# Attention and two expert layers in one kernel: rows turned earlier, rounding shared, and the last expert's width chosen at run time

## The chip, the cores and the metric

The kernel runs on one core of a Trainium2 chip. The metric is device time in microseconds (us), the median of 3 runs. The core has five instruction streams that work beside each other and meet at semaphores: TensorE (PE; its weight loads are listed as PEld), VectorE (DVE), ScalarE (ACT), GpSimd (POOL) and SyncE (SP), which issues most transfers.

## The reference, cut to what matters

```python
attn_out = _attn_ref(q, k, v)                    # 4 batches, 8 heads, 576 tokens, 64 wide, block-causal
x = attn_out.transpose(0, 2, 1, 3).reshape(B * S, H * D)     # 2304 tokens x 512
x = ((x @ w1) * (x @ w2)) @ w3 @ w_out                       # first expert layer, dense
logits = x @ w_gate                                          # second layer: each token picks 2 of 8 experts
noisy = logits + np.log1p(np.exp(x @ w_noise)) * noise
top2 = np.argpartition(-noisy, 2, axis=1)[:, :2]
for e in range(8):                                           # e_w1[e]: 512 x 1024, e_w2[e]: 1024 x 512
    h = np.maximum(x[mask] @ w1[e], 0.0)
    out[mask] += top2_w[mask, k, None] * (h @ w2[e])
```

The reference, evaluated on its own inputs (seed 0), gives the eight experts 607, 574, 540, 597, 592, 560, 591 and 547 rows.

## The kernel before, in words

Every float32 operand of a product is cut into a high part (rounded for TensorE) and a low part (what is left), and a product is made of three: high by high, low by high, high by low. ScalarE or GpSimd makes the high part, VectorE or GpSimd the low one.

The program has four phases: attention, the fusing of w3 and w_out, the dense layer with the choice of experts (`emit`), and the experts. Only the last and its seam are touched.

The experts' phase goes by **stretches** of at most 640 rows of one expert. Here each expert has one, so there are eight: the first is written out (`first_stretch`), the next six are turns of one loop (`Fori` in `through`), the last is written out again. A stretch has five tiles of 128 rows. For each, TensorE does this:

- **turn** a tile (`turn_x(g, j)`, L1573: four transposes of 128x128 out of `ex_rows` into the PSUM tile `ps_a`). ScalarE rounds the turned tile into `xT_high` (`high_x`, L1226), VectorE makes `xT_low` (`low_x`, L1341). There are two PSUM tiles for this (XS = 2), so the turn of tile j waits for `xT_low` of tile j-2.
- **first product** (`first_product(g, before, h, width)`, L1593): in two parts h of the rows. In the first stretch they are rows 0 to 383 and 384 to 639, later 0 to 255 and 256 to 639. Each part has 8 blocks of 12 matmuls (4 chunks, 3 products each). ScalarE makes `hT_high` with Relu, VectorE `hT_low`. In the six loop turns the second part is cut to the rows in use: 320, 352 or 384 columns, chosen from `widths_i` by three `pe.If` branches that stand one behind the other in the code. The last stretch always takes 384.
- **second product** (`second_product(g, before, j)`, L1617): per tile 24 matmuls of 128x512 into `ps_turn` or `ps_small`. VectorE scales the result into `y_tile` (`take_y`), and GpSimd sends it by an indirect accumulating transfer into `out` (`add_y`, L1196).

Weights of the next expert arrive in raw form by SP's queue (`spare` for the first matrix, `w_raw` for the second, 1 MB a piece, two pieces each). GpSimd cuts each piece into high (`cut_high`, L1148) and low (`cut_low`, L1154), and counts `weights_cut`; TensorE waits for 4 counts before the next stretch's first product, SP waits for the counts to load the next raw piece.

Only the first stretch has another order, since its rows come late. Tiles 0 to 2 (AHEAD = 3) are turned at the end of the dense layer; tiles 3 and 4 can only be loaded when the last rows have been scattered. Then `plan_experts` on VectorE computes the stretches, GpSimd's `know_rows` reads the token numbers and weights, and SP loads the next stretch's rows (`ex_rows`) behind four raw weight pieces (L1078) on its one queue. The order within each engine is the order in which its functions are written; semaphores alone tie the engines.

Of the kernel before, what the change touches and what calls it, by code (L numbers as in the profile page):

```python
# [5 lines left out]
F32 = mybir.dt.float32  # L6
F32R = mybir.dt.float32r
ALU = mybir.AluOpType
# [848 lines left out]
def gated_product_and_experts(nc, xT, parts, w_gate_noise, noise, consts, C, store, spare, ahead, plan, w1, w2, w1_raw, places):  # L857
# [30 lines left out]
    XS, HS, YS = 2, 4, 2  # L888
    CUTS = 2 * PIECES
    READS = 11  # L890

    with ExitStack() as ctx:  # L892
        def sb(name, shape, dt=F32):
# [96 lines left out]
        second_high = sem("second_high")  # L990
        second_low = sem("second_low")
        weights_cut = sem("weights_cut")
        x_loaded = [sem(f"x_loaded{j}") for j in range(TILES)]
        ex_turned = sem("ex_turned")
        xhigh = sem("xT_high_ready")
# [134 lines left out]
        def _(pool):  # L1130
# [60 lines left out]
            def add_y(g, j):  # L1191
                pool.wait_ge(y_taken, TILES * g + j + 1)
                if j == 0:
# [2 lines left out]
                nc.gpsimd.indirect_dma_start(out=out, out_offset=bass.IndirectOffsetOnAxis(ap=out_rows[:, j:j + 1], axis=0),  # L1196
                                             in_=y_tile[j][:], in_offset=None, compute_op=ALU.add).then_inc(y_added[j], 16)

            def stretch(g, before, last):
                if before is not None:  # L1200
                    pool.wait_ge(y_done, TILES * g)
                    for k in range(PIECES, 2 * PIECES):
                        cut_high(g, k)
                        cut_low(before, k)
                know_rows(g, before)
                if last:
                    for j in range(TILES):
                        add_y(g, j)
                    return
                pool.wait_ge(h_done, UNITS * (g + 1))  # L1210
                cut_high(g + 1, 0)
                cut_low(g, 0)
                add_y(g, 0)
                cut_high(g + 1, 1)
                add_y(g, 1)
                cut_low(g, 1)
                for j in range(2, TILES):
                    add_y(g, j)
# [4 lines left out]
        def _(act):  # L1223
# [16 lines left out]
            def first_stretch():  # L1240


                high_x(0, 2)
                route(GROUPS - 1, 2)
                route(GROUPS - 1, 3)
                second_high_part(0)
                high_h(0, 0, PARTS_FIRST)
                second_high_part(1)
                high_h(0, 1, PARTS_FIRST)
                route(GROUPS - 1, 5)  # L1250
                second_high_part(2)
                high_h(0, 2, PARTS_FIRST)
                second_high_part(3)
                for q in range(3, FC):
                    high_h(0, q, PARTS_FIRST)
                for j in range(AHEAD, TILES):
                    high_x(0, j)
                for q in range(FC, UNITS):
                    high_h(0, q, PARTS_FIRST)
                for j in range(TILES):  # L1260
                    high_x(1, j)

            def stretch(g, before, last):
# [69 lines left out]
        def _(dve):  # L1333
# [30 lines left out]
            def first_stretch():  # L1364
# [22 lines left out]
                    take_y(0, None, j)  # L1387
                for q in range(FC, UNITS):
                    low_h(0, q, PARTS_FIRST)
                take_y(0, None, AHEAD - 1)  # L1390
                for j in range(AHEAD, TILES):
                    take_y(0, None, j)
                    for k in (range(AHEAD) if j == AHEAD else range(AHEAD, TILES)):
                        low_x(1, k)

            def stretch(g, before, last):
# [141 lines left out]
        def _(pe):  # L1538
# [61 lines left out]
            def second_product(g, before, j):  # L1600
# [9 lines left out]
                for f in range(FC):  # L1610
                    for h in range(len(parts)):
                        if rows.start == parts[h].start:
                            pe.wait_ge(hlow, UNITS * g + FC * h + f + 1)
                    if before is None and j == 0 and f % (FC // QUARTERS) == 0:
                        pe.wait_ge(second_low, f // (FC // QUARTERS) + 1)
                    for lhsT, rhs in ((hT_high, ew2_high), (hT_high, ew2_low), (hT_low, ew2_high)):
                        mm = nc.tensor.matmul(ps_y[j % YS][:], lhsT[:, f, rows], rhs[:, f], start=(n == 0), stop=(n == 3 * FC - 1))  # L1617
                        n += 1
                    if before is None and j == 1 and f >= FC - (TILES - AHEAD):
                        turn_x(0, f - FC + TILES)  # L1620
                mm.then_inc(y_done, 1)

            def first_stretch():

                first_product(0, None, 0)
                second_product(0, None, 0)
                second_product(0, None, 1)
                first_product(0, None, 1)
                second_product(0, None, 2)
                second_product(0, None, 3)  # L1630
                for j in range(AHEAD):
                    turn_x(1, j)
                second_product(0, None, 4)
                for j in range(AHEAD, TILES):
                    turn_x(1, j)

            def stretch(g, before, last):
                if before is None:
                    return first_stretch()
                pe.wait_ge(weights_cut, 2 * CUTS * before + CUTS)  # L1640
                first_product(g, before, 0)
                if last:
                    first_product(g, before, 1)
                else:
                    step = pe.value_load(widths_i[0:1, bass.ds(g, 1)], min_val=0, max_val=len(WIDTHS) - 1)
                    for k, width in enumerate(WIDTHS):
                        with pe.If(step == k):
                            first_product(g, before, 1, width)
                pe.wait_ge(weights_cut, 2 * CUTS * before + 2 * CUTS)
                for j in range(TILES):  # L1650
                    second_product(g, before, j)
# [284 lines left out]
```

## Time and profile before

| | us |
|---|---|
| median of 3 runs | 1051.24 (1050.34 to 1051.44) |
| the profiled execution | 1052.73 |
| its span (first to last instruction) | 1050.6 |
| TensorE busy | 1019.5 (97% of the span) |
| GpSimd busy | 540.7 (51%) |
| VectorE busy | 443.0 (42%) |
| ScalarE busy | 365.1 (35%) |

A share of busy time is a mean over all phases. Whether one engine's wait costs anything is read from TensorE: it is idle in very few places, and each row below marked with `[idle before <-releaser]` is one of them. All times in rows are microseconds from the span's start.

### The profile page before, as it was taken

How to read it: one execution, taken by the hardware profiler on the slowest of the kernel's cores; microseconds unless marked ns; L12 is line 12 of the kernel's file. 1: busy time of each engine (PE TensorE's matmuls, PEld its weight loads, DVE VectorE, ACT ScalarE, POOL GpSimd, SP SyncE). 2: the span in 40 equal slices, each digit the busy share in tenths (PEclk: the TensorE clock that was granted, in tenths of full speed). 3: DMA queues.
4: the chain of work that ended last, by engine and by line, in shares of the span. 5: the costliest groups of instructions: out<-in, count | busy, mean ns of one | idle time of the engine just before them, and what ended most of it. 6: DMA issues, size and time to landing. Idle time of an engine off the chain costs nothing.

```text
span 1050.6 us, 16706 instructions
## 1 busy us (share of the span) xinstructions
PE 1019.5 (97%) x5927; PEld 937.4 (89%) x5928; DVE 443.0 (42%) x935; ACT 365.1 (35%) x679; POOL 540.7 (51%) x426
## 2 busy tenths in 40 slices
PE   7999999898999999999999999999999999999996
PEld 5999999787989898989898988889898989898995
DVE  5788888664224243333325742222222223222211
ACT  5999888753212232222223411212121212111110
POOL 8688899530000202020202229968778787878742
PEclk8999999999999999999999999999999999999998
DMA  8788887293970101010402165362717163634303
GB/s 168 169 199 191 202 205 175 69 269 100 369 281 2 60 0 60 0 60 0 140 1 85 48 250 126 92 167 67 192 37 213 20 195 65 190 70 140 41 4 47
DMA packets 73681, 125.25 MB, mean 119 GB/s; under 512 B 13073, under 2 KB 30609, under 8 KB 73634
## 3 DMA queue, kind: packets, MB, share of 16 engines
q1 hardware_dynamic: 64594, 103.74, 34.1%
q0 software_dynamic: 8960, 20.61, 9.9%
q8 instruction: 28, 0.46, 0.2%
q10 hardware_dynamic: 80, 0.29, 0.1%
q14 instruction: 19, 0.16, 0.1%
HBM read 78.73 MB, written 36.67 MB: 110 GB/s over the span
## 4 chain that ended last, share of the span: by engine, by line
PE 72%; POOL 1%; DVE 1%; issue 1%; ACT 0%; POOLq 0%; DVEq 0%
PE ps_turn L1617 11%; PE ps_b L1593 10%; PE ps_x L1593 10%; PE ps_a L1670 9%; PE ps_x L1688 9%; PE ps_b L1670 9%; PE ps_small L1617 8%; PE ps_a L1573 1%; PE ps_small L1565 1%; PE ps_turn L1555 1%; POOL w_high L1148 1%; POOL w_low L1154 1%; POOL out L1196 0%; PE ps_small L1547 0%; POOLq L892 0%
## 5 line engine op out<-in xcount | busy, mean ns | idle before, releaser
L1139 POOL DMA_INDIRECT expert_rows<-x_rows,slot_idx x36 | 41.7, 1159 | 307.5 <-DVE slot_idx L1493 298.4
L1196 POOL DMA_INDIRECT out<-y_tile,out_rows x40 | 63.3, 1581 | 77.1 <-DVE y_tile L1357 72.4
L1226 ACT CAST xT_high<-ps_a 128x512 fp32r<-128x512 f32 x40 | 23.3, 587 | 197.3 <-PE ps_a L1573 197.3
L1593 PE MATMUL ps_b<-xT_high,w_high 128*128 128x256 f32 (+3 forms) x256 | 78.0, 305 | 2.1 <-DVE xT_low L1341 1.4
L1294 ACT COPY prod<-ps_a 128x384 f32<-128x384 f32 x48 | 23.0, 479 | 163.7 <-PE ps_b L1670 163.7
L1500 DVE TENSOR_TENSOR prod<-ps_b,prod 128x384 f32<-128x384 f32 x48 | 26.7, 557 | 125.5 <-ACT prod L1294 125.5
L1617 PE MATMUL ps_turn<-wo_high,hT_high 128*128 128x512 f32 x192 | 76.2, 397 | 1.4 <-DVE hT_low L1348 1.4
L1593 PE MATMUL ps_x<-xT_high,w_high 128*128 128x256 f32 (+3 forms) x256 | 77.3, 302 | 0.0
L1593 PE MATMUL ps_x<-xT_high,w_low 128*128 128x256 f32 (+3 forms) x256 | 77.2, 302 | 0.0
L1593 PE MATMUL ps_x<-xT_low,w_high 128*128 128x256 f32 (+3 forms) x256 | 77.2, 302 | 0.0
L1593 PE MATMUL ps_b<-xT_high,w_low 128*128 128x256 f32 (+3 forms) x256 | 77.2, 302 | 0.0
L1593 PE MATMUL ps_b<-xT_low,w_high 128*128 128x256 f32 (+3 forms) x256 | 77.2, 302 | 0.0
L1617 PE MATMUL ps_turn<-wo_high,hT_low 128*128 128x512 f32 x192 | 75.0, 391 | 0.0
L1617 PE MATMUL ps_turn<-wo_low,hT_high 128*128 128x512 f32 x192 | 74.9, 390 | 0.0
L306 DVE TENSOR_TENSOR pT_low<-work,pT_high 128x512 fp32r<-128x512 f32 (+2 forms) x112 | 68.1, 627 | 11.1 <-ACT work L390 10.6
L1148 POOL TENSOR_TENSOR w_high<-spare,consts 128x2048 fp32r<-128x2048 f32 x14 | 54.3, 3882 | 33.0 <-PE ps_x L1593 33.0
L1670 PE MATMUL ps_a<-x_high,w_high 128*128 128x384 f32 x192 | 66.5, 347 | 2.8 <-DVE x_low L1527 2.8
L1154 POOL TENSOR_TENSOR w_low<-spare,w_high 128x2048 fp32r<-128x2048 f32 x14 | 68.4, 4888 | 0.5
L389 ACT ACTIVATE pT_high<-work 128x512 fp32r<-128x512 f32 (+2 forms) x112 | 62.1, 555 | 9.8 <-PE work L528 9.3
L1154 POOL TENSOR_TENSOR wo_low<-w_raw,wo_high 128x2048 fp32r<-128x2048 f32 x14 | 64.8, 4627 | 1.1
L1670 PE MATMUL ps_a<-x_high,w_low 128*128 128x384 f32 x192 | 64.9, 338 | 0.0
L1670 PE MATMUL ps_a<-x_low,w_high 128*128 128x384 f32 x192 | 64.8, 337 | 0.0
(269 smaller groups left out, 3024.4 us busy)
## 6 DMA issues: line engine op xcount, KB each, us to landing
spare<-e_w SPq DMA_DIRECT2D x16, 1024.0 KB, 5.2
w_raw<-e_w SPq DMA_DIRECT2D x16, 1024.0 KB, 8.7
expert_rows<-zeros SPq DMA_DIRECT2D x8, 1290.0 KB, 15.1
ex_rows<-expert_rows SPq DMA_DIRECT2D x40, 258.0 KB, 4.4
k_raw<-kT SPq DMA_DIRECT2D x31, 288.0 KB, 4.9
out<-zeros SPq DMA_DIRECT2D x11, 512.0 KB, 10.6
q_raw<-qT SPq DMA_DIRECT2D x16, 288.0 KB, 5.4
q_mix<-q_top SPq DMA_DIRECT2D x16, 288.0 KB, 3.8
```

The costliest lines, as they stand in the source:

```text
L306: nc.vector.tensor_tensor(unit_of(pT_low, unit), unit_scores(unit), unit_of(pT_high, unit).bitcast(F32), ALU.subtract)\
L389: nc.scalar.activation(unit_of(pT_high, unit), unit_scores(unit), ACT.Exp, scale=SCALE).then_inc(high_done, 1)
L1139: nc.gpsimd.indirect_dma_start(out=rows_dram, out_offset=bass.IndirectOffsetOnAxis(ap=slot_idx[:, k, t:t + 1], axis=0), in_=x_rows[:, t, : ...
L1148: nc.gpsimd.tensor_tensor(high, loaded, zero.unsqueeze(2).to_broadcast(list(loaded.shape)), ALU.add)\
L1154: nc.gpsimd.tensor_tensor(low, loaded, high.bitcast(F32), ALU.subtract).then_inc(weights_cut, 1)
L1196: nc.gpsimd.indirect_dma_start(out=out, out_offset=bass.IndirectOffsetOnAxis(ap=out_rows[:, j:j + 1], axis=0), in_=y_tile[j][:], in_offset ...
L1226: nc.scalar.copy(xT_high[:, :, j * P:(j + 1) * P], ps_xT[j % XS][:].rearrange("p (c t) -> p c t", t=P)).then_inc(xhigh, 1)
L1500: nc.vector.tensor_tensor(prod[f % 2][:], ps_b[f % 2][:, 0:G], prod[f % 2][:], ALU.mult).then_inc(prod_done, 1)
L1593: mm = nc.tensor.matmul(ps_hT[q % HS][:, 0:rows.stop - rows.start], lhsT[:, c, f * P:(f + 1) * P], rhs[:, c, rows], start=(n == 0), stop=( ...
L1617: mm = nc.tensor.matmul(ps_y[j % YS][:], lhsT[:, f, rows], rhs[:, f], start=(n == 0), stop=(n == 3 * FC - 1))
L1670: mm = nc.tensor.matmul(ps[f % 2][:, 0:G], lhsT[:, c, f * P:(f + 1) * P], rhs[:, c], start=(n == 0), stop=(n == 3 * DC - 1))
L1688: mm = nc.tensor.matmul(ps_x[t % 2][:], lhsT[:, f, t * P:(t + 1) * P], rhs[:, f], start=(n == 0), stop=(n == 3 * FC - 1))
```

## The change

Five edits, all in the experts' phase:

1. In the second product of tile 1 of the first stretch, the turns of tiles 3 and 4 stand behind blocks 3 and 4 (of 0 to 7), where they stood behind 6 and 7.
2. The five turns of the next stretch's tiles in the first stretch stand as 2, 2 and 1 behind the second products of tiles 2, 3 and 4; they stood as 3 and 2 behind tiles 3 and 4. VectorE's `low_x` follows the same table.
3. ScalarE rounds the two pieces of the next first weights, between the second and the third turned tile; GpSimd's two `cut_high` of that place are gone and it makes the low parts only.
4. GpSimd issues the output transfers of tiles 0 and 1 before these low parts, where the first stood behind the first piece and the second in the midst of the second.
5. The last stretch chooses its width by the same three branches as the loop turns.

```diff
+    LATE_TURNS = (3, 4)
+    NEXT_TURNS = {2: (0, 1), 3: (2, 3), 4: (4,)}
...
+            def first_stretch():                     # GpSimd
+                know_rows(0, None)
+                for j in range(AHEAD - 1):
+                    add_y(0, j)
+                for k in range(PIECES):
+                    loaded, high, low = piece(k)
+                    pool.wait_ge(next_high, k + 1)
+                    nc.gpsimd.tensor_tensor(low, loaded, high.bitcast(F32), ALU.subtract).then_inc(weights_cut, 2)
+                for j in range(AHEAD - 1, TILES):
+                    add_y(0, j)
...
-                for j in range(TILES):               # ScalarE
+                for j in NEXT_TURNS[AHEAD - 1]:
+                    high_x(1, j)
+                for k in range(PIECES):
+                    loaded, high, _ = piece(k)
+                    act.wait_ge(raw_loaded[k], 16)
+                    act.wait_ge(h_done, UNITS)
+                    nc.scalar.copy(high, loaded).then_inc(next_high, 1)
+                for j in range(len(NEXT_TURNS[AHEAD - 1]), TILES):
                     high_x(1, j)
...
-                take_y(0, None, AHEAD - 1)           # VectorE
-                for j in range(AHEAD, TILES):
+                for j in range(AHEAD - 1, TILES):
                     take_y(0, None, j)
-                    for k in (range(AHEAD) if j == AHEAD else range(AHEAD, TILES)):
+                    for k in NEXT_TURNS[j]:
                         low_x(1, k)
...
-                    if before is None and j == 1 and f >= FC - (TILES - AHEAD):     # TensorE
-                        turn_x(0, f - FC + TILES)
+                    if before is None and j == 1 and f in LATE_TURNS:
+                        turn_x(0, AHEAD + LATE_TURNS.index(f))
...
-                second_product(0, None, 2)
-                second_product(0, None, 3)
-                for j in range(AHEAD):
-                    turn_x(1, j)
-                second_product(0, None, 4)
-                for j in range(AHEAD, TILES):
-                    turn_x(1, j)
+                for j in range(AHEAD - 1, TILES):
+                    second_product(0, None, j)
+                    for k in NEXT_TURNS[j]:
+                        turn_x(1, k)
...
-                if last:
-                    first_product(g, before, 1)
-                else:
-                    step = pe.value_load(widths_i[0:1, bass.ds(g, 1)], min_val=0, max_val=len(WIDTHS) - 1)
-                    for k, width in enumerate(WIDTHS):
-                        with pe.If(step == k):
-                            first_product(g, before, 1, width)
+                step = pe.value_load(widths_i[0:1, bass.ds(g, 1)], min_val=0, max_val=len(WIDTHS) - 1)
+                for k, width in enumerate(WIDTHS):
+                    with pe.If(step == k):
+                        first_product(g, before, 1, width)
```

What this does to the streams is shown at three places. First GpSimd, from the end of `know_rows` (L1189) to the end of the first stretch; L1148 is a high part, L1154 a low part, L1196 an output transfer. Before:

```order
L1189 CAST out_rows<-row_of 128x5 [waits rows_read]
L1148 TENSOR_TENSOR w_high<-spare,consts 128x2048 [waits raw_loaded0,h_done]
L1154 TENSOR_TENSOR w_low<-spare,w_high 128x2048 [waits weights_cut]
L1196 DMA out<-y_tile_4238,out_rows 2944x512 [waits y_taken,rows_known]
L1148 TENSOR_TENSOR w_high<-spare,consts 128x2048 [waits raw_loaded1]
L1196 DMA out<-y_tile_4239,out_rows 2944x512 [waits y_taken]
L1154 TENSOR_TENSOR w_low<-spare,w_high 128x2048 [waits weights_cut]
L1196 DMA out<-y_tile_4240,out_rows 2944x512 [waits y_taken]
```

And now (L1199 is the transfer, L1210 the low part):

```order
L1192 CAST out_rows<-row_of 128x5 [waits rows_read]
L1199 DMA out<-y_tile_4238,out_rows 2944x512 [waits y_taken,rows_known]
L1199 DMA out<-y_tile_4239,out_rows 2944x512 [waits y_taken]
L1210 TENSOR_TENSOR w_low<-spare,w_high 128x2048 [waits next_high] x2
L1199 DMA out<-y_tile_4240,out_rows 2944x512 [waits y_taken]
```

The two high parts have left this stream, the first two transfers no longer wait for the first product's end (h_done), and the other three still stand behind both low parts.

Second, ScalarE at the same place, now (before, one row `xT_high<-ps_a` x5 stood where the last four rows stand; L1248 is `high_h`, L1242 `high_x`, L1282 the new rounding):

```order
L1248 ACTIVATE hT_high<-ps_b 128x256 [waits h_done] x2
L1248 ACTIVATE hT_high<-ps_x 128x256 [waits h_done] x2
L1242 CAST xT_high<-ps_a 128x4x128 [waits ex_turned] x2
L1282 CAST w_high<-spare 128x2048 [waits h_done,raw_loaded0]
L1282 CAST w_high<-spare 128x2048 [waits h_done,raw_loaded1]
L1242 CAST xT_high<-ps_a 128x4x128 [waits ex_turned] x3
```

The third turned tile now queues behind both roundings.

Third, TensorE. The end of the second product of tile 1 (`ps_small`, three matmuls to a block) before, with the first product's second part behind it:

```order
L1617 MATMUL ps_small<-wo_high,hT_low 128x512
L1573 MATMUL ps_a<-consts,ex_rows 128x128 x4
L1617 MATMUL ps_small<-wo_high,hT_high 128x512
L1617 MATMUL ps_small<-wo_low,hT_high 128x512
L1617 MATMUL ps_small<-wo_high,hT_low 128x512
L1573 MATMUL ps_a<-consts,ex_rows 128x128 x4
L1593 MATMUL ps_b<-xT_high,w_high 128x256
```

Now the same two turns have a block between them and more of the second product behind:

```order
L1595 MATMUL ps_a<-consts,ex_rows 128x128 x4
L1639 MATMUL ps_small<-wo_high,hT_high 128x512
L1639 MATMUL ps_small<-wo_low,hT_high 128x512
L1639 MATMUL ps_small<-wo_high,hT_low 128x512
L1595 MATMUL ps_a<-consts,ex_rows 128x128 x4
L1639 MATMUL ps_small<-wo_high,hT_high 128x512
```

And the end of the narrowest branch of the last stretch, now (before, this part was straight code of 96 matmuls of 128x384):

```order
L1615 MATMUL ps_x<-xT_high,w_high 128x320
L1615 MATMUL ps_x<-xT_high,w_low 128x320
L1615 MATMUL ps_x<-xT_low,w_high 128x320
L1663 UNCONDITIONAL_BRANCH
L1663 COMPARE_AND_BRANCH
L1601 REGISTER_ALU
L1605 REGISTER_ALU
L1615 MATMUL ps_b<-xT_high,w_high 128x352
```

Behind it stand the 96 matmuls of 352 columns and the 96 of 384, each jumped over when not chosen, and then the second product.

## Rows read from the trace of the kernel before

**Rows 1.** Waits of TensorE, 570 to 1051 us (line, releaser: total us, times, longest).
```profile
PE ps_b L1593 <- DVE xT_low L1341: 1.4, 1, 1.4
PE ps_turn L1617 <- DVE hT_low L1348: 1.4, 1, 1.4
PE ps_a L1573 <- DVE xT_low L1341: 1.1, 1, 1.1
```

**Rows 2.** Timeline of TensorE around the late turns: start, us, instruction, [idle before].
```profile
608.48 0.39 PE L1617 MATMUL ps_small<-wo_high,hT_high 128*128 128x512 f32 x1
...
614.37 0.60 PE L1573 MATMUL ps_a<-consts,ex_rows 128*128 128x128 f32 x4
616.37 0.39 PE L1593 MATMUL ps_b<-xT_high,w_high 128*128 128x256 f32 x1 [1.40 <-DVE xT_low L1341]
```

**Rows 3.** Timeline of TensorE at the end of the first stretch.
```profile
633.46 0.39 PE L1617 MATMUL ps_small<-wo_high,hT_high 128*128 128x512 f32 x1
...
638.90 1.04 PE L1573 MATMUL ps_a<-consts,ex_rows 128*128 128x128 f32 x8
640.99 0.63 PE L1573 MATMUL ps_a<-consts,ex_rows 128*128 128x128 f32 x4 [1.05 <-DVE xT_low L1341]
641.38 0.48 PE L1617 MATMUL ps_turn<-wo_high,hT_high 128*128 128x512 f32 x1
...
648.64 0.38 PE L1593 MATMUL ps_b<-xT_high,w_high 128*128 128x256 f32 x1 [0.67 <-POOL w_low L1154]
```

**Rows 4.** Timeline of GpSimd, 631 to 649 us.
```profile
631.92 4.61 POOL L1154 TENSOR_TENSOR w_low<-spare,w_high 128x2048 fp32r<-128x2048 f32 x1
...
643.24 5.15 POOL L1154 TENSOR_TENSOR w_low<-spare,w_high 128x2048 fp32r<-128x2048 f32 x1
```

**Rows 5.** ScalarE's casts by form (count, busy us, mean ns, idle before).
```profile
L760 ACT CAST w_high<-spare 128x1024 fp32r<-128x1024 f32 x8 | 8.4, 1052 | 1.8 <-DMA spare<-w 1.8
...
L1322 ACT CAST x_high<-xT 128x1536 fp32r<-128x1536 f32 x1 | 1.5, 1476 | 0.0
```

**Rows 6.** Issues in windows 606.9:608, 618:618.2, 636:637 (count, KB, us to landing).
```profile
ex_rows<-expert_rows SPq DMA_DIRECT2D x2, 258.0 KB, 2.9
...
ex_rows<-expert_rows SPq DMA_DIRECT2D x1, 258.0 KB, 9.5
...
out<-y_tile,out_rows POOLq DMA_INDIRECT x1, 6.5
```

**Rows 7.** Windows (busy per engine, PEclk); the last two columns are DMA share and GB/s.
```profile
616.00:618.00 2.00, 1.63 (x13) 1.63 (x14) 1.63 (x3) 0.00 (x0) 0.00 (x0) 1.00 1.02 418
...
642.00:648.00 6.00, 5.97 (x31) 4.80 (x29) 1.44 (x2) 0.67 (x2) 5.83 (x3) 1.00 0.45 62
```

**Rows 8.** Chain that ended last, whole span: start, us, what.
```profile
616.37 3.14 PE ps_b L1593 x24
...
657.53 2.88 PE ps_x L1593 x24
660.41 3.52 PE ps_b L1593 x24
...
670.97 3.53 PE ps_x L1593 x24
675.84 5.74 PE ps_turn L1617 x24
...
727.76 3.52 PE ps_x L1593 x24
731.28 5.47 PE ps_turn L1617 x24
...
1009.36 4.16 PE ps_x L1593 x24
1013.52 5.48 PE ps_turn L1617 x24
```

**Rows 9.** DMA queues, window 672:674 (queue: packets, MB, share).
```profile
q8 instruction: 1, 0.02, 4.2%
```

More of the change, by code:

```diff
@@ L992, in gated_product_and_experts @@
         weights_cut = sem("weights_cut")
+        next_high = sem("next_high")
         x_loaded = [sem(f"x_loaded{j}") for j in range(TILES)]
@@ L1197, in add_y @@
                                              in_=y_tile[j][:], in_offset=None, compute_op=ALU.add).then_inc(y_added[j], 16)
-            def stretch(g, before, last):
[L1200 to L1204, printed above, removed]
+            def first_stretch():
[8 more added lines that the diff above has]
+                    add_y(0, j)
+            def stretch(g, before, last):
+                if before is None:
+                    return first_stretch()
+                pool.wait_ge(y_done, TILES * g)
+                for k in range(PIECES, 2 * PIECES):
+                    cut_high(g, k)
+                    cut_low(before, k)
                 know_rows(g, before)
```

## Prediction

> **What bounds the kernel now.** I read the waits first. In the experts' phase TensorE is idle at four places that concern this change [rows 1, 3]; elsewhere its matmuls follow one another, and over the whole span it is busy for 97% (the page's table). So a gain must be one of these waits, or fewer columns on TensorE. Then I read the timelines around each wait, to see who ends it and who comes next, then the other engines and the queues there, and last the chain through the second, the third and the last stretch.
>
> The waits: (a) 1.40 us before 616.37, where the first product's second part waits for `xT_low` of tile 4, turned just before [rows 2]; (b) 1.05 before 640.99, where the third turn in a row waits for a PSUM tile [rows 3]; (c) 0.67 before 648.64, where the second stretch waits for GpSimd's last low part [rows 3]; (d) 1.34 between 674.50 (670.97 + 3.53) and 675.84, before the second product of the second stretch [rows 8]. The profile puts (d) down to `hT_low`, but the second product of tile 0 needs only the first part's rows, whose `hT_low` is long done. It occurs in the first loop turn alone: in the next one 727.76 + 3.52 = 731.28 is exactly where the second product starts [rows 8]. In the window just before it a packet of instructions is fetched [rows 9]. I read (d) as code that had not arrived: after the 320-column branch the program jumps over two bodies of 96 matmuls each.
>
> **Edit 1, the late turns.** Before, the last late turn starts at 614.37 and the product that needs it at 616.37: the way turn, ScalarE, VectorE, TensorE takes 2.00 us [rows 2]. A second product of 24 matmuls takes 638.90 - 633.46 = 5.44 us [rows 3], so a block of three takes 0.68. The second product of tile 1 starts at 608.48 [rows 2]; the first late turn now starts after four blocks, at 611.2, the second after one turn (0.44: four transposes of the eight in 1.04, less the overlap) and one block, at 612.3, and its result is usable at 614.3. TensorE ends this second product at 614.97 as before (614.37 + 0.60). So (a) goes whole, 1.40. What could be late instead is the rows: tiles 3 and 4 come by two issues near 607 that land after 2.9 us, at 609.9 [rows 6], and the turn comes 1.3 us later. A product that starts after a wait also fills slowly: the first 24 matmuls took 3.14, unbroken ones 2.88 [rows 8], so 0.26 more. I count 1.66; bounds 0 (the rows late by that much) and 1.66.
>
> **Edit 2, the next turns.** No more than two turns stand together, so none waits for a PSUM tile: (b) goes, 1.05. One more change between kinds of matmul costs 0.48 - 0.39, about 0.1, the first matmul behind a turn against one in the row [rows 3]. The turns are five, as before.
>
> TensorE's new calendar, if nothing waits: the first product's second part from 614.97, four times 2.88, to 626.5; second product of tile 2 to 632.0; two turns to 632.9; tile 3 to 638.4; two turns to 639.3; tile 4 to 644.9; one turn to 645.35. Then the next stretch starts, if its weights are cut.
>
> **Edits 3 and 4, the weights.** GpSimd's second low part ended at 643.24 + 5.15 = 648.39 [rows 4], and TensorE started 0.25 behind it. Now ScalarE rounds the first two turned tiles (from 632.0, done at 633.7) and then the two pieces. The trace has no ScalarE cast of 128x2048. 128x1024 took 1.052 and 128x1536 took 1.476 [rows 5]; on that line 2048 columns take 1.90. Bounds: 1.5 (no shorter than 1536 columns) and 2.1 (twice 1024). GpSimd starts its first low part at 635.6, takes 4.61, and the second ends at 644.85; with 5.15 for each [rows 4] it ends at 645.9. TensorE wants it at 645.35. So (c) goes, 0.67 and the slow fill 0.26, together 0.93, less 0 to 0.8. What is late next is this same low part, by a margin of nothing. Queued behind the two roundings on ScalarE is the third turned tile: ScalarE is free again at 637.5, and that tile is turned only at 638.4. VectorE's `low_x` and `take_y` have TensorE's calendar, and TensorE needs them next for the turn of tile 4 at 644.9. Queued behind the low parts on GpSimd are the transfers of tiles 2 to 4, which leave from 645 on where they left from 648.4 on: nobody waits longer. SP loads the next raw piece into `spare` behind the first low part, at 640.2 instead of 636.5 (631.92 + 4.61), and GpSimd reads it only when the second stretch's first product is through, past 670: hidden.
>
> Moved past others are the two output transfers. They now go out at 616 to 618 and meet SP's queue, where four raw pieces and then the rows of the next stretch are under way with all 16 DMA engines full (share 1.02, 418 GB/s) [rows 7]. The first tile of these rows is issued at 618.1 and lands 9.5 us later, at 627.6 [rows 6]. It was wanted at 638.9 and is now wanted at 632.0: the slack falls from 11.3 to 4.4. An output transfer issued at 642.2 stands nearly alone in the window 642 to 648, 0.45 x 6 = 2.7 us of all engines [rows 7]. Two are 5.4: in the worst order tile 0 lands at 633.0 and tile 1 some 0.8 later, wanted at 632.4, a wait of up to 1.4. In the best order they take nothing that the rows need: 0. I take 0.2 for this and for the margin above together.
>
> The DMA page says that each DMA engine goes round between the queues it has work for, packet by packet (Trainium skill, DMA: Bandwidth & Descriptors, Queues, rings and completion order). By that rule the two transfers get through beside SP's queue, what they take falls on what is last there, the rows, and the sum would be 1.2 us smaller than mine; no row here shows the two together.
>
> **Edit 5, the width.** The last expert has 547 rows by the reference, so 320 columns. In the last stretch 24 matmuls of 384 columns take 4.16, in the loop 24 of 320 take 3.52 [rows 8]; there are four such groups, 4 x 0.64 = 2.56 less. But this code was straight: the second product started without a gap, at 1009.36 + 4.16 = 1013.52 [rows 8]. Now it has the loop's jumps, in code met for the first time. The one first time that the trace shows is (d): 1.34, and a slow restart of 5.74 - 5.47 = 0.27 [rows 8]. It is the same branch, 320 columns with two bodies jumped, so I charge 1.61. Bounds: 0 (the code is there) and 3.2 (both jumps wait). The load of the width's register in the second stretch cost nothing: 657.53 + 2.88 = 660.41 is where the part begins [rows 8]. ScalarE and VectorE get the loop's pace, and the last transfers follow TensorE's end as before.
>
> The launch page says that a taken jump whose target is outside the fetched window forces a fetch before execution goes on (Trainium skill, Runtime: NRT & Kernel Launch, Instruction fetch mechanics). The trace agrees in (d). The page also says that only straight fetching is served, by which every loop turn would pay; the third stretch pays nothing [rows 8], and there the trace decides.
>
> **The sum.** First stretch: 1.66 + 1.05 - 0.10 + 0.93 - 0.20 = 3.34. Last: 2.56 - 1.61 = 0.95. Together 4.3. Against the profiled execution, 1052.73 - 4.3 = 1048.4; that one lies 1.5 above the median of the runs. For the median: 1051.24 - 4.3 = **1046.9**. The gap (d) itself stays: as many instructions stand ahead of it as before.
>
> **Rivals.**
>
> *The branch is free.* If the fetched code is already there, the last stretch keeps its 2.56: 1046.9 - 1.6 = 1045.3. For it: the third stretch jumps without a gap. Against it: its code had run before.
>
> *The branch gives nothing.* Each of the two jumps waits in full, 3.2 against 2.56: 1051.24 - 3.34 + 0.65 = 1048.6. For it: two jumps, each to code not yet run. Against it: in (d) two jumps cost 1.6 together. The launch page's rule, taken jump by jump, is this case.
>
> *The rows or the low part are late.* 1.4 us at the turn or 0.8 at the low part, of which 0.2 is counted: 1047.5 to 1048.1. For it: full DMA engines and a margin of nothing. Against it: 4.4 us of slack.
>
> *Slower.* The mechanism is the two early output transfers. They read and add in memory; if, on full engines, they go one after the other and hold up the rows for their whole time to landing, 6.5 us each as the one of 636.7 [rows 6], the first tile lands at 627.6 + 13 = 640.6. Its turn is 8.6 late, the second stretch starts at 645.35 + 8.6 = 654.0 instead of 648.64, and with 0.95 from the last stretch the kernel takes 1051.24 + 5.3 - 0.95 = 1055.6. It decides once the rows are delayed by more than 4.4 + 3.3 + 0.95 = 8.6 us. Against it: 2.7 us of engine time each.
>
> **Chances.** Forecast 0.55; branch free 0.14; branch gives nothing 0.09; rows or low part late 0.14; slower 0.04; all else 0.04. A measurement of this kernel can tell about 0.2%, 2.1 us, from no change, so faster means below 1049.1: the first four, less the cases where two losses meet, 0.88. Within 0.2%: 0.08. Slower: 0.04. The range, 1045.0 to 1049.4, holds the first four with their unknown costs and leaves out the slower case.
>
> **What would show it.** Right: no wait at the start of the first product's second part near 615, none between turns; the second stretch starting near 645.3 instead of 648.64, with a few tenths at most waited for the low part; ScalarE's new casts near 1.9 each; 24 matmuls of 320 columns in 3.52 in the last stretch, and 1.3 to 1.4 us of gap before its second product. Wrong: a turn that waits for `ex_rows` near 632, the second stretch starting after 647, or a gap in the last stretch of nothing or near 3.

## The result, and the profile after

| | before | after |
|---|---|---|
| median of the runs | 1051.34 us (1050.34 to 1052.70, 4 runs) | 1045.44 us (1044.77 to 1045.93, 4 runs) |
| ratio | | 0.9937, 95% interval 0.9919 to 0.9954 |
| profiled execution (span) | 1052.73 (1050.6) | 1045.19 (1043.0) |

By the ratio the kernel is faster by 6.6 us (4.8 to 8.5), where 4.3 were forecast; the two medians differ by 5.9. The ratio times 1051.24 is 1044.6, just under the low end of the range, 1045.0.

The two spans differ by 7.6 us. The first stretch's first product starts at 585.82 before and at 584.67 after, so 1.15 us lie in phases that the change does not touch. That start fell anywhere between 582.6 and 589.8 us in the kernels below. I therefore measure every kernel from that start, by the starts of TensorE's matmuls in its timeline. A runs from there to the second stretch's first product; B from there to its second product; C is the same as B in the last stretch; "all" is the way to the last matmul.

| kernel | A | B | C | all |
|---|---|---|---|---|
| before | 62.82 | 27.20 | 28.23 | 454.56 |
| after | 59.10 | 27.09 | 25.67 | 448.14 |
| after less before | -3.72 | -0.11 | -2.56 | -6.42 |

Of the waits at [rows 1, 3], the two for `xT_low` and the one for GpSimd's `w_low` are gone. The one put down to `hT_low` stays. Waits of TensorE after the change, 570 to 1051 us (columns as in rows 1):

```profile
PE ps_turn L1639 <- DVE hT_low L1371: 1.2, 1, 1.2
PE ps_small L1587 <- DVE w_raw L1545: 0.8, 1, 0.8
PE ps_turn L1577 <- ACT x_rows L1339: 0.2, 1, 0.2
```

The timeline of TensorE after the change answers to [rows 2, 3]: the two late turns, the first product's second part, the first two next turns and what follows them, the start of the second stretch.

```profile
610.05 0.60 PE L1595 MATMUL ps_a<-consts,ex_rows 128*128 128x128 f32 x4
...
611.19 0.60 PE L1595 MATMUL ps_a<-consts,ex_rows 128*128 128x128 f32 x4
...
613.72 0.28 PE L1615 MATMUL ps_b<-xT_high,w_high 128*128 128x256 f32 x1
...
630.69 1.03 PE L1595 MATMUL ps_a<-consts,ex_rows 128*128 128x128 f32 x8
631.48 0.48 PE L1639 MATMUL ps_small<-wo_high,hT_high 128*128 128x512 f32 x1
...
643.77 0.38 PE L1615 MATMUL ps_b<-xT_high,w_high 128*128 128x256 f32 x1
```

No bracket stands behind any of these: TensorE is never idle before them. The second part now starts 613.72 - 584.67 = 29.05 behind A's start; before it was 616.37 - 585.82 = 30.55. The second stretch starts at 643.77, which on the clock of before (1.15 later) is 644.92, where 645.35 was forecast. Two turns take 631.48 - 630.69 = 0.79 from start to start. Before, the two turns with the wait (b) behind them took 640.99 - 638.90 = 2.09 [rows 3], so (b) had cost 1.30: its 1.05 and a slow restart of 0.25.

ScalarE and GpSimd after the change, in the same stretch, answer to [rows 4]:

```profile
632.29 3.73 ACT L1282 CAST w_high<-spare 128x2048 fp32r<-128x2048 f32 x2
...
615.82 1.70 POOL L1199 DMA_INDIRECT out<-y_tile,out_rows  x1 [1.71 <-DVE y_tile L1380]
617.83 1.58 POOL L1199 DMA_INDIRECT out<-y_tile,out_rows  x1 [0.31 <-issue]
634.36 9.17 POOL L1210 TENSOR_TENSOR w_low<-spare,w_high 128x2048 fp32r<-128x2048 f32 x2 [14.95 <-ACT w_high L1282]
```

The two casts take 1.87 each and the two low parts 9.17 together. GpSimd ends at 643.53, and TensorE starts 0.24 later. Before, where it did wait for the low part, it started just as long behind it (648.39 and 648.64). So the margin of nothing that was forecast is what the trace shows, and yet no wait is seen.

The chain of waits after the change, in the second and in the last stretch (start, us, what), answers to [rows 8]:

```profile
666.10 3.53 PE ps_x L1615 x24
...
670.86 5.74 PE ps_turn L1639 x24
...
1002.46 3.52 PE ps_x L1615 x24
1005.98 5.46 PE ps_turn L1639 x24
```

In the second stretch 666.10 + 3.53 = 669.63, and the second product starts 1.23 later. In the last one 1002.46 + 3.52 = 1005.98 is exactly where the second product starts. The width branch runs there at the pace of 320 columns, and the gap that I had charged for it is not there.

### The profile page after: what moved, and what is told of

It is laid out like the page before. It is cut to its first block, busy times and chain, and to the rows that moved or that the text cites. A ratio compares the mean times of both kernels' runs of the same rounds, so it can differ in the third digit from the quotient of the medians.

```text
span 1043.0 us, 16716 instructions
## 1 busy us (share of the span) xinstructions
PE 1014.5 (97%) x5927; PEld 933.6 (90%) x5928; DVE 443.0 (42%) x935; ACT 368.3 (35%) x681; POOL 533.9 (51%) x424
## 4 chain that ended last, share of the span: by engine, by line
PE 74%; DVE 1%; ACT 0%; POOLq 0%; issue 0%; DVEq 0%
PE ps_turn L1639 13%; PE ps_x L1615 10%; PE ps_b L1615 10%; PE ps_a L1686 10%; PE ps_x L1704 9%; PE ps_b L1686 9%; PE ps_small L1639 8%; PE ps_a L1595 2%; PE ps_small L1587 1%; PE ps_turn L1577 1%; PE ps_small L1569 0%; POOLq L894 0%; PE ps_small L1570 0%; DVE y_tile L1380 0%; DVE w_raw L1545 0%
## 5 line engine op out<-in xcount | busy, mean ns | idle before, releaser
L1199 POOL DMA_INDIRECT out<-y_tile,out_rows x40 | 63.3, 1581 | 76.1 <-DVE y_tile L1380 71.5
L1242 ACT CAST xT_high<-ps_a 128x512 fp32r<-128x512 f32 x40 | 23.3, 587 | 190.3 <-PE ps_a L1595 190.3
L1686 PE MATMUL ps_b<-x_high,w_high 128*128 128x384 f32 x192 | 64.4, 335 | 0.0
L1686 PE MATMUL ps_b<-x_low,w_high 128*128 128x384 f32 x192 | 64.3, 335 | 0.0
```

Of the source, the lines that this page charges most:

```text
L1242: nc.scalar.copy(xT_high[:, :, j * P:(j + 1) * P], ps_xT[j % XS][:].rearrange("p (c t) -> p c t", t=P)).then_inc(xhigh, 1)
L1686: mm = nc.tensor.matmul(ps[f % 2][:, 0:G], lhsT[:, c, f * P:(f + 1) * P], rhs[:, c], start=(n == 0), stop=(n == 3 * DC - 1))
```

## The experiments

The first stretch first, then the code fetch. The whole time of a single execution is of little use (the phases ahead scatter by more than the effects), so what is said of each kernel rests on A, B and C of one trace; only the changed kernel, no_branch and pad_both have a ratio of several runs too. A short table at the end has them all.

**late_only.** Before, with the two late turns as changed.

```diff
-                    if before is None and j == 1 and f >= FC - (TILES - AHEAD):
-                        turn_x(0, f - FC + TILES)
+                    if before is None and j == 1 and f in LATE_TURNS:
+                        turn_x(0, AHEAD + LATE_TURNS.index(f))
```

> The kernel before with edit 1 alone (late turns behind blocks 3 and 4). Theory: the wait of 1.40 us before the first product's second part goes with its slow fill, and GpSimd's cuts, which start at the end of that product, start as much earlier. From the first stretch's first product to the second stretch's it is 62.67 us before; expected 61.0 (1.66 less). Waits of 1.05 (third turn) and about 0.7 (low part) stay. Rival (the rows of tiles 3 and 4 or GpSimd hold it up): nothing gained, 62.7.

A is 61.20, 1.62 less than before, against a term of 1.66. The other two waits of the first stretch stand as they were, in the waits of TensorE of this kernel:

```profile
PE ps_a L1575 <- DVE xT_low L1343: 1.1, 1, 1.1
PE ps_turn L1619 <- issue: 1.0, 1, 1.0
...
PE ps_b L1595 <- POOL w_low L1156: 0.7, 1, 0.7
```

The term of edit 1 is as forecast. The gap (d) is in the list too, 1.0 long, and here the profile names no releaser for it but "issue".

**turns_only.** The late turns and the spread next turns (edits 1 and 2), with the weights and the transfers as before.

```diff
+    NEXT_TURNS = {2: (0, 1), 3: (2, 3), 4: (4,)}
```

> The kernel before with edits 1 and 2 (late turns, next turns spread), the weights cut by GpSimd with the transfers in between as before. My prediction's terms were added up: by them 62.67 - 1.66 - 1.05 + 0.10 = 60.06 us from first product to first product. Theory now: GpSimd's second low part is the bound (it ended at 648.39 and is only 1.66 earlier), so 61.0, with the wait for the low part grown to about 1.6; edit 2 alone gains nothing.

A is 61.17: the spread turns add 0.03 to edit 1 alone, although the wait between turns is gone. The waits of TensorE in this kernel:

```profile
PE ps_b L1594 <- POOL w_low L1156: 1.9, 1, 1.9
```

What was waited for a PSUM tile is now waited for GpSimd: 0.7 has become 1.9. GpSimd's calendar hadn't moved, and TensorE merely came earlier to the same release.

**no_scalar.** After, without ScalarE's rounding: GpSimd rounds and subtracts itself, as before, but with the two transfers ahead of all its pieces (edit 3 undone, edit 4 kept).

```diff
+                pool.wait_ge(h_done, UNITS)
                 for k in range(PIECES):
-                    pool.wait_ge(next_high, k + 1)
-                    nc.gpsimd.tensor_tensor(low, loaded, high.bitcast(F32), ALU.subtract)...
+                    cut_high(1, k)
+                    cut_low(0, k)
```

> The changed kernel with edit 3 undone: GpSimd cuts both pieces itself (high and low), but the first two transfers stay ahead and nothing lies between the cuts. Theory: what freed the path is the two transfers' removal, not ScalarE's rounding. GpSimd starts at the end of the first product and takes 3.60 + 4.61 + 3.60 + 4.61 and small gaps, 16.6 us, so it ends 2 us before TensorE's second stretch wants it: 59.15 us from first product to first product as in the changed kernel, no wait for the low part. Rival (ScalarE's rounding is needed): GpSimd's parts take 4.2 and 5.2 as in the crowded place, 18.8 us, and TensorE waits 0.3 to 1.

A is 59.07, the same as after within 0.03. Timeline of GpSimd in this kernel:

```profile
627.72 3.60 POOL L1151 TENSOR_TENSOR w_high<-spare,consts 128x2048 fp32r<-128x2048 f32 x1 [6.03 <-PE ps_x L1610]
631.39 4.61 POOL L1157 TENSOR_TENSOR w_low<-spare,w_high 128x2048 fp32r<-128x2048 f32 x1
...
639.63 4.60 POOL L1157 TENSOR_TENSOR w_low<-spare,w_high 128x2048 fp32r<-128x2048 f32 x1
```

GpSimd alone ends at 639.63 + 4.60 = 644.23; TensorE starts the second stretch at 646.00 in this kernel, so the low part ends 1.8 ahead of that, where ScalarE's help leaves 0.2. From the start of the first piece to the end of the last GpSimd takes 644.23 - 627.72 = 16.51 here; before, with two output transfers between the pieces, it took 648.39 - 628.24 = 20.15. These 3.6 us had made it late. Given edit 4, edit 3 takes nothing off the time, and it narrows the margin. Edit 3 with the transfers in their old places was not run.

**no_spread.** After, with the turns where they were before.

```diff
-    NEXT_TURNS = {2: (0, 1), 3: (2, 3), 4: (4,)}
+    NEXT_TURNS = {2: (), 3: (0, 1, 2), 4: (3, 4)}
```

> The changed kernel with edit 2 undone: the next turns stand as 3 and 2 again, ScalarE rounds the pieces ahead of all of them. Theory: the wait of 1.05 us for a PSUM tile at the third turn is back, 60.1 us from first product to first product (59.15 + 1.05 - 0.10). Rival (the wait was only the other side of GpSimd's lateness): 59.2.

A is 60.60, 1.50 more than after. The wait between turns is back with 1.06, and with it 0.25 of slow restart: from the two turns to the third it is 641.34 - 639.24 = 2.10 on TensorE's timeline, against 0.79 for two turns without a wait. The other 0.2 lies just ahead of the second stretch and stays open. So edit 2 is worth 1.5 with edits 3 and 4 in place, and 0.03 without them. By no_scalar edit 4 is the one of the two that counts: edits 2 and 4 are one gain that needs both parts.

**transfers_late.** After, with all five output transfers behind the low parts.

```diff
-                for j in range(AHEAD - 1):
-                    add_y(0, j)
...
-                for j in range(AHEAD - 1, TILES):
+                for j in range(TILES):
                     add_y(0, j)
```

> The changed kernel with edit 4 undone, farther than before: all five output transfers stand behind both low parts (ScalarE still rounds). Theory: the two transfers cost the next rows 2.8 us (time to landing of the first 9.5 again, where the changed kernel has 12.3), but the rows are not waited for, so 59.1 us from first product to first product as in the changed kernel. Rival (my prediction's, that the transfers can hold up the turn): shorter than 59.1.

A is 59.09, as after. What counts is that no transfers stand between GpSimd's pieces; whether they leave early or last is the same. They do take the rows' time. Issues of DMA in this kernel, window 621:622.2 (count, KB, us to landing):

```profile
ex_rows<-expert_rows SPq DMA_DIRECT2D x1, 258.0 KB, 9.4
```

And the issues of the same rows in the changed kernel, window 616:617.2:

```profile
ex_rows<-expert_rows SPq DMA_DIRECT2D x1, 258.0 KB, 12.3
out<-y_tile,out_rows POOLq DMA_INDIRECT x1, 9.4
```

Two transfers among the full queues delay the first tile of rows by 2.9 us; their engine time, twice 2.7, had bounded it at 5.4. The rows land at 629.2 and are turned at 630.69: of the slack 1.5 is left. The Trainium skill says that each DMA engine takes the queues that have work in turn, packet by packet (DMA: Bandwidth & Descriptors, Queues, rings and completion order). The trace agrees in so far as the transfer gets through beside SP's full queue, in 9.4 us, and the rows issued at about the same time land 2.9 us later than those of the transfers_late kernel.

**early_turns and early_turns_late.** These use the slack up. The first two next turns stand ahead of the second product of tile 2 instead of behind it, 5.5 us earlier, and VectorE's low parts of these tiles go with them; in the second kernel the transfers are late as well.

```diff
                 for j in range(AHEAD - 1, TILES):
+                for k in NEXT_TURNS[AHEAD - 1]:
+                    turn_x(1, k)
...
                     second_product(0, None, j)
-                    for k in NEXT_TURNS[j]:
+                    for k in NEXT_TURNS[j] if j >= AHEAD else ():
                         turn_x(1, k)
```

> The changed kernel with the first two next turns ahead of the second product of tile 2, 6.4 us earlier. The rows land at about 629.3 (first tile) and 629.8 on the changed kernel's clock, where the turn would now come at 625.4: TensorE waits 3.9 to 4.5 us, and about 63.2 us lie from first product to first product (59.1 + 4.1). This shows how near the changed kernel is to the edge: its slack to the rows is 1.5 us. Rival (rows are there when the product ends, since the landing times overstate): 59.2.

> As early_turns, with all output transfers behind the low parts. Here the rows bind, so the price of edit 4 shows as time: the first tile lands 2.8 us earlier, TensorE waits 1.1 to 1.7, and 60.4 us lie from first product to first product. Rival (the transfers go beside the rows without cost): the same as early_turns.

A is 66.00 and 62.23, both more than I expected (63.2 and 60.4). In early_turns the wait for the rows was 3.5 us, and then something came that no term of mine had. Chain of waits of early_turns:

```profile
628.11 1.97 PE ps_a L1597 x8
630.08 7.33 PE ps_turn L1641 x24
637.41 5.45 PE ps_small L1641 x24
```

Windows of early_turns (busy time and count of PE, PEld, DVE, ACT and POOL, then PEclk, DMA share, GB/s):

```profile
624.00:628.00 4.00, 0.59 (x5) 0.38 (x4) 0.46 (x2) 0.38 (x1) 0.00 (x0) 0.89 1.05 363
628.00:630.00 2.00, 1.89 (x9) 1.89 (x10) 0.12 (x1) 0.59 (x1) 0.00 (x0) 0.50 0.80 305
...
634.00:636.00 2.00, 2.00 (x10) 1.63 (x10) 0.00 (x0) 0.30 (x1) 2.00 (x1) 1.00 0.00 0
```

After TensorE had stood almost idle for 3.5 us, its granted clock was 0.50, the 1.2 GHz level, from 628 to about 634. The first product of 24 took 7.33 where the next took 5.45, 1.9 more. Eight transposes took 1.97, against 1.03 without a wait and 1.34 behind the short wait of early_turns_late, so 0.6 of it goes with the clock. That is 2.5 us on top of the wait. With the transfers late the wait was 1.1, and the clock stayed at 1.00. Windows of early_turns_late, the wait at the end of the first:

```profile
622.00:626.00 4.00, 3.10 (x26) 2.90 (x25) 1.27 (x3) 1.15 (x3) 0.00 (x0) 1.00 1.05 388
626.00:630.00 4.00, 3.78 (x20) 3.08 (x21) 1.37 (x2) 3.02 (x4) 0.00 (x0) 1.00 0.22 82
```

So where the rows are needed, the two early transfers cost 66.00 - 62.23 = 3.8 us of A. Up to the last turn of the first stretch it is more, 65.16 - 60.22 = 4.9, of which 2.4 is waiting (3.5 less 1.1) and 2.5 goes with the clock. A shows less of it because early_turns_late has one more wait behind that turn: 1.4 ahead of the second stretch, put down to `xT_low`. That name can't be the reason. The part that starts there needs `xT_low` of tiles 0 and 1 only, which VectorE had done by 628.9, and the weights were cut at 639.3, both long before 646.64; nor does a packet of TensorE's instructions move between 633 and 654. What it waits for stays open.

**no_branch.** After, with the last stretch's first product straight and 384 wide again (edit 5 undone).

```diff
-                step = pe.value_load(widths_i[0:1, bass.ds(g, 1)], ...)
-                for k, width in enumerate(WIDTHS):
+                if last:
+                    first_product(g, before, 1)
+                else:
```

> The changed kernel with the last stretch's first product in straight code of 384 columns (edit 5 undone). If edit 5 gained its full 2.56 us in the changed kernel, the last stretch takes 2.5 to 2.6 us more from the start of its first product to the start of its second; everything ahead of it as in the changed kernel, the second stretch starting 3.6 us earlier relative to the first than before. Ratio to the kernel before about 0.9965 (0.997 if only the forecast's 3.3 us are there).

C is 28.23, exactly as before, so the branch is worth 2.56 in C, which is four groups of 0.64 with no gap. The whole way is 450.88 against 448.14, 2.74 more, of which 0.16 is in B. The timed ratio to before is 0.9965 (0.9946 to 0.9984), median 1048.14 of 10 runs. That is worse than the changed kernel's 0.9937, though the two intervals overlap; that the branch is faster rests on the way on TensorE.

**pad_small, pad_loop, pad_last, pad_both.** If (d) is code that had not arrived, it should depend on where the code lies and not on `hT_low`. These kernels add instructions that are never run and are jumped over: ahead of the loop over the stretches, or in the last stretch ahead of its first product, or both.

```diff
             if engine is pads_in[0]:
+                with engine.If(last == 0):          # ahead of the loop: 80
+                    for _ in range(80):
+                        engine.sem_inc(waited, 1)
...
                 if last:
+                    with pe.If(g == 0):             # last stretch: 170, 60 or 5
+                        for _ in range(170):
+                            pe.sem_inc(waited, 1)
```

pad_both has both (80 and 170), pad_loop only the first, pad_last only the second with 60, pad_small only the second with 5.

> As pad_last, the same extra jump in front of the last stretch, but over 5 instructions instead of 60. Theory (code fetch by position): in the changed kernel the second product's code lies some 20 to 30 instructions ahead of the edge of its block, so 5 and the two of the jump leave it inside, and no gap appears in the last stretch. Rival (it is the extra jump that costs, not the position): a gap of 0.9 us as in pad_last.

> The changed kernel with 60 TensorE instructions that are never run in front of the last stretch only. Theory (code fetch by position): the second product's code moves into the next block of 256, which is asked for only at the jump, and a gap of 1.2 to 1.6 us (with 0.27 of slow restart) appears before the last stretch's second product, at the place where the changed kernel has none; the gap in the second stretch stays at 1.2. Rival (a first pass through a branch costs nothing, the gap in the second stretch has another cause): no gap in the last stretch.

> The changed kernel with 80 TensorE instructions that are never run in front of the loop. Theory (code fetch by position): the gap in the second stretch goes and one of 1.2 to 1.6 us appears in the last stretch, so the total is as in the changed kernel. Rival (the gap is a wait for data): the gap in the second stretch stays, none appears in the last.

> The changed kernel with two blocks of TensorE instructions that are never run (jumped over): 80 in front of the loop over stretches, 170 in front of the last stretch. Theory (code fetch by position): the gap of 1.23 us before the second stretch's second product, and its slow restart of 0.27, go, since the code at the far side of the jumps was asked for more than 4 us earlier; no gap appears in the last stretch. From the start of the first stretch's first product to the end of the last second product 1.5 us less than the changed kernel; ratio to the kernel before about 0.992. Rival (the gap is a wait for hT_low, or for weights, as the profile names it): the gap stays at 1.2, ratio as for the changed kernel, 0.994.

pad_small changes nothing (C 25.67). So one more jump costs nothing that can be seen. With 60 instead of 5 instructions to jump over, a gap appears in the last stretch; chain of waits of pad_last:

```profile
1002.36 3.52 PE ps_x L1615 x24
1005.88 0.91 issue
1006.79 5.27 PE ps_turn L1639 x22
```

C is 26.74, 1.07 more. pad_loop, with 80 ahead of the loop, does both things at once. B falls to 25.69: the gap (d) is gone. And C rises to 27.03. Its chain of waits:

```profile
664.90 3.37 PE ps_x L1621 x23
668.27 5.47 PE ps_turn L1645 x24
...
1003.14 0.02 issue
1003.16 0.50 ACT hT_high L1254
1003.66 0.02 issue
1003.68 0.57 DVE hT_low L1377
1004.25 0.07 issue
1004.32 5.73 PE ps_turn L1645 x24
```

In the second stretch 664.90 + 3.37 = 668.27: no gap. In the last one there is 1.18 from 1003.14 to 1004.32, and the chain draws it as a way over ScalarE and `hT_low`. In the changed kernel the same code, with the same data and the same `hT_low`, started without a wait. So the releaser's name in (d) is a coincidence of times, and the position of the code decides. pad_both puts both places right; its chain of waits in the second and in the last stretch:

```profile
664.70 3.52 PE ps_x L1621 x24
668.22 5.47 PE ps_turn L1645 x24
...
999.55 3.52 PE ps_x L1621 x24
1003.07 5.46 PE ps_turn L1645 x24
```

664.70 + 3.52 = 668.22 and 999.55 + 3.52 = 1003.07: no gap anywhere. B is 25.69, C 25.67, the whole way 446.63, 1.51 less than after. It takes 1043.64 us (1042.28 to 1045.76, 6 runs), a ratio to before of 0.9915 (0.9899 to 0.9932). It is the best version that ran, by the way on TensorE; by the timed ratios alone its interval overlaps with the changed kernel's.

| kernel | A | B | C | all |
|---|---|---|---|---|
| late_only | 61.20 | 26.85 | 28.23 | 452.57 |
| turns_only | 61.17 | 27.02 | 28.23 | 452.73 |
| no_scalar | 59.07 | 27.25 | 25.68 | 448.27 |
| no_spread | 60.60 | 27.46 | 25.67 | 450.00 |
| transfers_late | 59.09 | 26.85 | 25.67 | 448.13 |
| early_turns | 66.00 | 26.86 | 25.67 | 454.81 |
| early_turns_late | 62.23 | 27.22 | 25.67 | 451.41 |
| no_branch | 59.11 | 27.25 | 28.23 | 450.88 |
| pad_small | 59.14 | 26.86 | 25.67 | 448.18 |
| pad_last | 59.09 | 27.43 | 26.74 | 449.63 |
| pad_loop | 59.09 | 25.69 | 27.03 | 448.09 |
| pad_both | 59.10 | 25.69 | 25.67 | 446.63 |

B scatters by 0.6 as long as the gap is in it, 26.85 to 27.46, and not at all without it (25.69 twice). With the branch and without a gap, C is 25.67 or 25.68 in all eight kernels, the changed one among them.

## Why the prediction was right and wrong

**Edit 1, 1.66.** Right: 1.62 alone. The rows of tiles 3 and 4 were there in time.

**Edit 2, 1.05 - 0.10.** The wait went as forecast, but not as a term by itself: on top of edit 1 alone it gives 0.03, since the low part is next. I had listed the low part's margin under the weights and not as what caps this edit. The sum was saved because edit 4 is in it. And the term was too small: I had given the waits (a) and (c) a slow restart and this one none, where (b) had cost 1.30 and not 1.05.

**Edits 3 and 4, 0.93 less 0 to 0.8.** The durations were right (1.87 for 1.90; 9.17 for 9.2), and so was the release, at a margin of nothing. The credit was wrong: edit 4 does it without edit 3, and ScalarE's rounding takes 1.5 us of margin away. I had never worked out what GpSimd would do without the transfers between its pieces. The 0.20 set aside for rows and low part was not used. The whole first stretch gave 3.72 for 3.34: these 0.20 and the 0.25 of (b), less 0.07 of small ones.

**The transfers' price.** Bounds of 0 and 5.4, measured 2.9, with 1.5 of slack left. Nobody waits for the rows, as forecast. The rival "slower" was not near. The slack of 4.4 less these 2.9 is the 1.5 that is left, and that is thin: a turn 5.5 us earlier loses 3.5 us of waiting and 2.5 more with the clock. My price for the case that the rows pay for both transfers was 1.2 us more. They did pay, but 2.9 and not 5.4, so nothing was lost.

**The gap (d) stays.** Right: 0.11 less, within its scatter. That it is code and not `hT_low` is shown by pad_loop and pad_both. The reason that I gave for its staying (as many instructions ahead of it) was half of the truth: it is the position that counts, and 80 instructions were enough to remove it.

**Edit 5, 2.56 - 1.61.** This is the step that failed. The 2.56 is exact. The 1.61, charged as the price of meeting the loop's jumps in new code, was not paid at all, and the rival "the branch is free" came true. I had taken the one first pass that the trace showed as what each first pass costs. It is a price that depends on where the target lies: zero in the changed kernel, and in C 1.07 with 60 instructions more, 1.36 with 80 more ahead of the loop. Where it is paid, its size was right: on the whole way it is 448.09 - 446.63 = 1.46 for pad_loop against pad_both, and 1.51 for (d). My bounds, 0 and 3.2, held the truth, but no row before the change said which value it would be, so 14 in 100 for a free branch against 55 for a paid one rested on (d) alone. That this layout of the code pays nothing is luck: 60 instructions more lose 1.07 of the 2.56 (pad_last).

The difference, 6.42 against 4.3 forecast, is thus 1.61 of edit 5, 0.38 of the first stretch, 0.11 of (d) and 0.03 at the end. By the ratio the kernel gained 6.6, 0.2 more than this, which is inside the interval.

## What to carry to other kernels

Before adding up the waits that edits remove, ask for each what would release TensorE next: two edits may be worth 1.5 together and 0.03 apart, and a third, made with them, nothing. A wait that occurs only in the first pass through a piece of code, and that is put down to an engine long done, is to be tried with instructions ahead of it that are never run; if it moves or goes, it is code. Slack towards a DMA is to be known before it is used: a wait of 3.5 us on TensorE cost 2.5 more with its clock, while one of 1.1 left the clock at 1.00.

## What the runs showed of the hardware

*Code and jumps.* Each packet on the instruction queue q8 moves 0.02 MB. It moved 28 packets before, 29 after the change with its two more bodies of 96 matmuls, and 30 in pad_last, pad_loop and pad_both, whose additional instructions are TensorE's alone. Just ahead of (d) in the changed kernel, in the window 667:668 of its queues (queue: packets, MB, share):

```profile
q8 instruction: 1, 0.02, 7.4%
```

By windows of 0.05 us that packet moves at 667.95, and the second product starts at 670.86, 2.9 later. Before, it is 672.80 and 675.84, so 3.0; ahead of the gap in the last stretch it is 1004.15 and 1006.79 in pad_last, so 2.6, and 1001.40 and 1004.32 in pad_loop, so 2.9. In pad_both, which has no gap, the packet comes in the window 660:662, 6 us or more ahead of the product at 668.06:

```profile
q8 instruction: 1, 0.02, 2.7%
```

No instruction packet moves between 681.8 and 982.0, while the loop goes round: its turns run from what is there. The Trainium skill says that a taken jump whose target is outside the fetched pages stalls until the page is there (Runtime: NRT & Kernel Launch, Instruction fetch mechanics); the first passes agree, with gaps of 0.9 to 1.6 us. It says there as well that the instruction memory is only two cache lines and that fetching ahead is purely sequential; the loop, whose first turn drew four packets from 652 to 682 us and whose later ones none, disagrees. Which distances stall, these few positions don't say; that stays open.

*The clock.* After 3.5 us of idleness TensorE came back at a granted clock of 0.50, the 1.2 GHz level, and stayed there for some 6 us (early_turns). After 1.1 it came back at 1.00 (early_turns_late).

*Transfers that add.* Two of 128 rows, among full queues, held back by 2.9 us the rows that were issued beside them, and landed after 9.4 us, where one nearly alone took 6.5 [rows 6].
